# Two score steps side by side at the head of each attention half, with the first two groups of a hidden layer behind both

## The reference

```python
def reference(**kwargs):
    attn_out = _attn_ref(r, k, v, w, u)      # linear attention with decay: 8 heads of 48, state carried over tokens
    x = attn_out.transpose(0, 2, 1, 3).reshape(B, S, H * D)                 # 4 x 768 x 384
    x = _moe_ref(x, w_gate, wq, wk, wv, wo)
    return _moe2_ref(x, mu_k, mu_r, w_k, w_v, w_r)

# _moe_ref, for each of 4 experts e (head size 64), causal softmax attention, gated by the top 2 of 4:
    scores = scale * (q @ k.transpose(0, 2, 1)); scores[causal] = -1e9
    a = np.exp(scores - scores.max(-1)); a /= a.sum(-1) + 1e-9
    out += gate_e * (a @ v @ wo[e])
# _moe2_ref, the mixing layer:
    xk = mu_k * x + (1 - mu_k) * x_prev;  xr = mu_r * x + (1 - mu_r) * x_prev
    k = np.maximum(xk @ w_k, 0.0)            # hidden width 1024
    v = k * k @ w_v
    return sigmoid(xr @ w_r) * v
```

## Time and profile before

| | |
|---|---|
| median of 3 runs | 703.1 us (702.91 to 703.39) |
| the profiled execution: its own time, its span | 703.36 us, 701.6 us |
| mean granted TensorE clock | 0.995 of full speed |
| busy, share of the span | PE 97%, PEld 64%, DVE 55%, ACT 46%, POOL 22% |
| DMA | 43.37 MB, most of it in the first tenth of the span |

### The profile page before, as it was taken

How to read it: one execution, slowest core, us unless ns; L and a number is a source line. 1 busy time by engine, 2 the same in 40 slices (tenths; PEclk the granted TensorE clock), 3 DMA queues, 4 the chain that set the end, 5 groups by cost and what they waited for, 6 DMA issues and landing times.

```text
span 701.6 us, 12410 instructions
## 1 busy us (share of the span) xinstructions
PE 683.9 (97%) x4864; PEld 448.6 (64%) x4864; DVE 385.7 (55%) x753; ACT 320.9 (46%) x805; POOL 153.7 (22%) x199
## 2 busy tenths in 40 slices
PE   7969999999999999999999999999999999999998
PEld 7856666666656665666656665666665666566554
DVE  7897986382854656537463738637476223551200
ACT  2454566522662266622655227662175314563340
POOL 7772530053201601017010522004320000000000
PEclk9998999999999999999999999999999999999999
DMA  9996500004400080000800044000000000000000
GB/s 230 298 348 182 171 14 1 1 1 127 140 1 1 24 242 2 1 1 24 242 2 1 1 119 147 2 1 1 35 1 2 1 23 12 1 1 12 23 0 35
DMA packets 36922, 43.37 MB, mean 62 GB/s; under 512 B 2560, under 2 KB 27264, under 8 KB 36608
## 3 DMA queue, kind: packets, MB, share of 16 engines
q1 hardware_dynamic: 36864, 42.57, 20.8%
HBM read 37.84 MB, written 4.72 MB: 61 GB/s over the span
## 4 chain that ended last, share of the span: by engine, by line
PE 93%; DVE 3%; ACT 1%; POOL 1%; issue 1%; DVEq 0%; POOLq 0%; ACTq 0%
PE bank L924 81%; PE bank L928 6%; PE bank L1087 3%; PE bank L1083 3%; DVE idec L652 1%; DVE att L713 0%; ACT k_sb L442 0%; ACT shared L460 0%; DVE nmax L680 0%; DVE shared L693 0%; POOL rk_sb L345 0%; ACT shared L451 0%; DVE dec L644 0%; DVE cmp L761 0%; POOL rk_sb L343 0%
## 5 line engine op out<-in xcount | busy, mean ns | idle before, releaser
L924 PE MATMUL bank<-wv_sb,k_sb 128*128 128x384 f32 x384 | 139.4, 497 | 0.0
L924 PE MATMUL bank<-xk_sb,wk_sb 128*128 128x384 f32 x384 | 138.1, 499 | 0.0
L924 PEld LDWEIGHTS bank<-xk_sb,wk_sb 128*128 128x128 f32 x384 | 68.4, 190 | 42.9 <-issue 5.5
L924 PEld LDWEIGHTS bank<-wv_sb,k_sb 128*128 128x128 f32 x384 | 67.5, 190 | 38.8 <-issue 3.7
L652 DVE RECIPROCAL idec<-dec 112x260 f32<-112x260 f32 x48 | 82.8, 1755 | 0.5
L451 ACT ACTIVATE shared<-bank,nmax 128x128 f32<-128x128 f32 (+5 forms) x96 | 59.9, 629 | 47.3 <-DVE nmax L680 47.3
L680 DVE TENSOR_REDUCE nmax<-bank 128x1 f32<-128x128 f32 (+5 forms) x96 | 55.4, 619 | 46.7 <-PE bank L924 46.7
L376 POOL TENSOR_TENSOR state<-state,carry 112x512 f32<-112x512 f32 x20 | 22.0, 1099 | 260.1 <-DVE state L732 133.4
L924 PE MATMUL bank<-xT_sb,wqk_sb 128*128 128x384 f32 (+1 forms) x240 | 64.1, 424 | 0.6 <-ACT xT_sb L498 0.6
L481 ACT ACTIVATE att<-ident,bonus 128x128 f32<-128x128 f32 x192 | 58.0, 391 | 13.7 <-DVE bonus L660 10.7
L673 DVE TENSOR_TENSOR out_sb<-bank,sg_sb 128x384 f32<-128x384 f32 x24 | 13.4, 557 | 85.2 <-PE bank L924 84.9
(11 more groups left out here) (91 smaller groups left out, 922.2 us busy)
## 6 DMA issues: line engine op xcount, KB each, us to landing
rk_sb<-in_rk SPq DMA_DIRECT2D x24, 384.0 KB, 7.1
v_sb<-in_v SPq DMA_DIRECT2D x24, 256.0 KB, 7.5
w_sb<-in_wT SPq DMA_DIRECT2D x24, 227.5 KB, 4.8
r_sb<-in_rT SPq DMA_DIRECT2D x24, 224.0 KB, 5.1
k_sb<-in_kT SPq DMA_DIRECT2D x24, 224.0 KB, 6.3
out<-out_sb SPq DMA_DIRECT2D x24, 192.0 KB, 1.9
wk_sb<-in_w_k SPq DMA_DIRECT2D x1, 1536.0 KB, 12.3
wv_sb<-in_w_v SPq DMA_DIRECT2D x1, 1536.0 KB, 16.1
```

The costliest lines, as they stand in the source:

```text
L924: return nc.tensor.matmul(out, lhsT, rhs, start=start, stop=stop)
```

## The change

Two things are moved in the softmax half, for every `h` from 1 to 7. PE computes the scores of steps 0 and 1 directly behind each other and then groups 0 and 1; before, it was scores 0, group 0, scores 1, group 1. Since `fill_a` serves ACT too, ACT now takes out both groups after the exponentials of step 1. And banks: group 1 goes to bank 6 and not 7 (except in the last mixing layer, which has its own ring), and the sigmoid's third chunk to bank 6 and not 3 in every half. The waits follow the banks.

```diff
 def mix_bank(hh, i):
     if i < FT and hh != LAST:
-        return 7
+        return 6 if i == 1 else 7
 def r_bank(h, t):
-    return (4, 5, 6 if h == LAST else 3)[t]
+    return (4, 5, 6)[t]
 def fill_a(i):
-    groups = {0: ((0,), ()), 1: ((1,), ()), 2: ((), (2,)), 3: ((), (3,)), 4: ((), (4,)), 5: ((), (5,)), 6: ((6,), (7,))}[i]
+    groups = {0: ((), ()), 1: ((0, 1), ()), 2: ((), (2,)), 3: ((), (3,)), 4: ((), (4,)), 5: ((), (5,)), 6: ((6,), (7,))}[i]
...
+                    elif hidden and i == 1:
+                        pe.wait_ge(r_ready, (hh + 1) * HC)
                     elif hidden and i > 0:
-                        pe.wait_ge(relu_ready, hh * FT + i)
+                        pe.wait_ge(relu_ready, hh * FT + (i if i > 2 else 1))
...
-                if i == 1 and h > 0:
-                    pe.wait_ge(r_ready, h * HC)
...
                 elif h == 0:
                     pe.wait_ge(ktok_ready, NC - 1)
+                else:
+                    pe.wait_ge(relu_ready, (h - 1) * FT + 2)
...
                     if c == 2 and h < LAST:
-                        pe.wait_ge(proj_dve, h * (QM + HC) + 1)
+                        pe.wait_ge(proj_dve, h * (QM + HC) + QM + 1)
```

## The result

The changed kernel takes 705.06 us (median of 22 runs), the kernel before 703.32 in the same series: a ratio of 1.0025, 95% interval 1.0018 to 1.0032. It is 1.8 us slower, where 1.6 was forecast. The profiled execution took 704.73 us with a span of 703.0, against 703.36 and 701.6 before.

The account below looks back on a forecast made before the run. PE was taken to bound the kernel; 1.48 us (odd halves) and 0.15 (even halves) sum to +1.6, which on a median of 703.1 gives 704.7 us, eight-in-ten range 703.7 to 705.5.

Parts of the forecast that it names:

- What bounds the kernel: PE, busy 97% of the span: moving matmuls saves only changeovers and waits, and can lose by a new wait.
- ACT's Relu as the price: Odd halves: group 0's Relu, now behind step 1's exponentials, delays copies and first output by 0.37 us each, 1.48 in all.
- The even halves: From scores 0 to first output: ACT's hole takes group 0's Relu, so copy and output move 0.05 us each, 0.15 in all.
- DVE's order as the reason why nothing is won: Step 0's scaling stands ahead of step 1's maxima on DVE, so ACT's exponentials of step 1 don't start earlier.
- The edits costed at nothing: Sigmoid's third chunk's wait (about 4.9 us cover), moved waits, and scores 2 of odd halves (0.2 us spare) cost nothing.
- The changeover on PE: Groups 0 and 1 side by side: one changeover between kinds of matmul gone, saving about 0.12 us per half.
- the gain on offer: Changeovers in seven halves plus the bank stall in three even ones: 1.1 us, if nothing else moves.
- The signs that it named: New profile: adjacent Relus about 7.0 us after odd halves' first scores, ACT idle 2.1, PE waiting about 0.5, stretches 9.28 and 6.79.
- The slower and the half-hidden rival: Slower: a second wait in odd halves, +3.3 us, chance 0.05; half-hidden: half the odd term absorbed, +0.8, chance 0.14.

Follow-up runs that it names:

- experiment 5: Changed kernel, with ACT taking group 0's Relu once more into a spare tile ahead of it, in halves 1 to 7: 707.69 us, ratio 1.0064.
- experiment 1: Changed kernel, with ACT alone back on its old list (group 0's Relu ahead of step 1's exponentials): 702.78 us, ratio 0.9992.
- experiment 2: Kernel before in PE's order, with the new banks and ACT's new list (both Relus behind step 1's exponentials): 705.33 us, ratio 1.0028.
- experiment 3: Kernel before with only the new banks and their waits, PE's and ACT's orders as before: 703.02 us, ratio 0.9995.
- experiment 4: Changed kernel, with DVE taking step 1's maxima directly behind step 0's, ahead of gate weights and scaling: 702.27 us, ratio 0.9985.
- experiment 6: Kernel before, with groups 2 and 3 ahead of the outputs of steps 2 and 3 in even halves: 702.13 us, ratio 0.9978.

## Why the prediction was right

The forecast of +1.6 us stands against 1.7 (medians) or 1.8 (ratio), and 704.7 us against 705.06; 0.2 of the 0.36 between these two is that the kernel before took 703.32 in this series and not 703.1.

**What bounds the kernel** held: PE's matmuls are the same, and 1.7 of the 1.8 us are stretches that got longer, each by PE's wait at its first `output`.

**ACT's Relu as the price** held as a mechanism and in size. 0.37 us were forecast for each odd half; h=1 shows 0.37 and h=3 0.38, and the doubled cost of experiment 5 gives the same again. That the Relu was free in its old place is shown by experiment 1, and that its new place brings the loss whatever PE's order by experiment 2.

**The even halves** were forecast at +0.05 and show +0.06, by the forecast's own steps: the first Relu starts 0.09 us behind the read of the row sum, and the copy starts 194.10 - 187.74 = 6.36 us after scores 0, where it was 6.32. Behind that small number stand two parts: 0.16 us won by the bank of group 1 (6.74 to 6.58, experiment 3), and 0.21 lost to the Relu (6.58 to 6.79, experiment 3 against 2). The prediction had about 0.1 for the bank; it counted the stall and not that a group takes 190.95 to 192.99 = 2.04 us behind the stall, where it takes 2.00 in experiment 3. ACT's copies hide the difference.

**DVE's order as the reason why nothing is won** held: the start of the exponentials of step 1 did not move (5.65 us), and it moved 2.25 us earlier when DVE's list was changed (experiment 4).

**The edits costed at nothing** cost nothing. In experiment 3, which holds the banks with the waits for the first values' copy and for the second Relu, no window is longer. It doesn't hold group 1's wait for the sigmoids; that one is in the changed kernel itself, where behind 104 us PE shows no wait but those for the copies. Scores 2 of h=3 come 0.25 us behind the exponentials that they need (273.61 against 273.16 + 0.20), where 0.2 was forecast.

**The changeover on PE** was mis-sized. The prediction took 0.12 us a half for it, net, and named scores 1 behind scores 0's mask as not shown. The trace after shows it: scores 0 now take 267.54 - 266.26 = 1.28 us and not 1.18, so 0.10 is paid there. The two groups take 272.65 - 268.72 = 3.93 and not 2.09 + 1.99 = 4.08, so 0.15 is won. The net 0.05 agrees with experiment 4 in h=3, 8.85 against 8.91. The prediction counted one changeover gone; in fact one from a group to scores and one from scores to a group are gone, and one between two scores is new. So the gain on offer was 7 x 0.05 + 3 x 0.16 = 0.83 us and not 1.1. In the changed kernel all of it went into the waits, so the sum did not feel it: that this error cost the forecast nothing is owed to the copies being the bound.

**The signs that it named** came: in h=3 the Relus start 273.25 - 266.26 = 6.99 us after scores 0 (7.0), ACT idles 2.15 us ahead of the exponentials of step 1 (2.1), and the stretches are 9.29 and 6.80 us (9.28 and 6.79). PE's added wait at `output` is 0.65 - 0.22 = 0.43 us and not 0.49, since PE came 0.05 us earlier and not 0.12. **The slower and the half-hidden rival** did not: each odd half lost the full Relu and no more.

## What to carry to other kernels

When two pieces of work are moved together on the bounding engine, ask what the engines that serve it do with their own lists: here one helper gave PE's order and ACT's order, and ACT's part of the move took an instruction out of a hole of 1.8 us and put it into a place without slack. Being early is worth nothing past an engine whose list holds the next piece back; find that engine by following the late instruction, not the early one. And where PE stands at a copy for 0.2 us, look for independent matmuls to place ahead of that consumer: here six such moves, of two microseconds of matmuls each, took all the waits away (experiment 6). A faster copy was not tried.

## What the runs showed of the hardware

What a piece of work costs PE depends on what comes behind it. All times here are from start to start, at full clock, in stretches without a wait.

- A group (six records of 384 columns) takes 2.09 us in h=3 when scores follow and 1.99 when transposes follow. Twelve records in a row ahead of transposes take 3.93, which is 1.97 for six, as in the run of 18 of the earlier trace rows. So going from a group to scores costs about 0.12 us, and to transposes 0.02 at most.
- Scores of 512 columns with their mask take 1.18 us when a group follows and 1.28 when other scores follow. The difference lies behind the small bf16 mask matmul: from its start it is 0.12 or 0.13 us to a group (268.60 to 268.72; 194.81 to 194.94 in experiment 6), and 0.22 to scores (267.32 to 267.54) or to `output` (274.82 to 275.04 in the earlier trace rows).

Scores and `output` have 64 rows or 64 columns of weights where a group has 128 by 128. A group and the transposes, between which the change costs next to nothing, are both 128 by 128. Whether that is the reason is left open: no run changes it alone.
